# The third batch's norms and scatters a round sooner, both early tiles transposed together, the last batch counted sooner, and the next expert's reads behind the early tiles

## The reference

```python
# 1: gated linear attention, q, k, v, alpha: (4, 8, 768, 48)
for t in range(S):
    state = alpha[:, :, t, :, None] * state + np.einsum('bhd,bhe->bhde', k[:, :, t], v[:, :, t])
    y[:, :, t] = np.einsum('bhd,bhde->bhe', q[:, :, t], state)
x = y as 3072 tokens of 384
# 2: mixture of 8 experts, top 1; w1: (8, 384, 1024), w2: (8, 1024, 384)
logits = (x / (norm(x) + 1e-6)) @ (emb / (norm(emb) + 1e-6)).T / tau
gate_w = softmax(logits) at expert_idx = argmax(logits)
out[mask] = gate_w[mask, None] * (np.maximum(x[mask] @ w1[e], 0.0) @ w2[e])     # for each expert e
# 3: dense network, w_in: (384, 2048), w_out: (2048, 384)
h = x @ w_in
y = np.where(h > 0, h, np.exp(np.minimum(h, 0)) - 1) @ w_out
```

## Time and profile before

| | us |
|---|---|
| median of 3 runs | 927.77 |
| lowest, highest | 925.91, 928.4 |
| profiled execution, own time | 922.87 |
| its span | 921.2 |
| TensorE busy | 886.1 |
| VectorE busy | 435.5 |
| ScalarE busy | 321.7 |
| GpSimd busy | 273.0 |

### The profile page before, as it was taken

How to read it: one execution, slowest core, us unless ns; L and a number is a source line. 1 busy time by engine, 2 the same in 40 slices (tenths; PEclk the granted TensorE clock), 3 DMA queues, 4 the chain that set the end, 5 groups by cost and what they waited for, 6 DMA issues and landing times. The chain is left out here.

```text
span 921.2 us, 16309 instructions
## 1 busy us (share of the span) xinstructions
PE 886.1 (96%) x5729; PEld 779.3 (85%) x5729; DVE 435.5 (47%) x837; ACT 321.7 (35%) x708; POOL 273.0 (30%) x277
## 2 busy tenths in 40 slices
PE   7999999968999999999998999999999999999995
PEld 4777788757989899898997899999999999989994
DVE  6788787863222322223224545445445445445442
ACT  3556656622222222223222223223233223323221
POOL 2212444643576555635816400101001001001001
PEclk8999999979999999999999999999999999999998
DMA  9877875558768797775815301001001001000000
GB/s 151 122 132 120 167 134 107 202 176 274 267 210 283 241 336 251 203 239 150 249 32 163 121 1 44 26 1 52 18 1 61 9 0 66 4 1 35 1 1 34
DMA packets 140975, 107.92 MB, mean 117 GB/s; under 512 B 103354, under 2 KB 129074, under 8 KB 140898
## 3 DMA queue, kind: packets, MB, share of 16 engines
q0 software_dynamic: 25696, 66.09, 22.7%
q1 hardware_dynamic: 115202, 40.79, 21.1%
HBM read 89.51 MB, written 17.35 MB: 116 GB/s over the span
## 5 line engine op out<-in xcount | busy, mean ns | idle before, releaser
L1379 POOL DMA_INDIRECT out<-of,idi x24 | 23.6, 984 | 370.2 <-DVE of L1465 305.5
L1199 PE MATMUL bank<-WX,hdTh 128*128 (+1 forms) x496 | 129.0, 341 | 2.8 <-DVE hdTl L1252 1.6
L1423 PE MATMUL bank<-xT_h,wi_h 128*128 128x512 f32 x288 | 114.1, 396 | 0.0
L1423 PE MATMUL bank<-xT_l,wi_h 128*128 128x512 f32 x288 | 113.6, 394 | 0.0
L1423 PE MATMUL bank<-xT_h,wi_l 128*128 128x512 f32 x288 | 113.3, 394 | 0.0
L1483 ACT ACTIVATE ee<-bank 128x512 f32<-128x512 f32 x96 | 57.5, 598 | 147.3 <-PE bank L1423 144.5
L1505 DVE TENSOR_SCALAR em<-ee 128x512 f32<-128x512 f32 x96 | 44.4, 462 | 136.4 <-ACT ee L1483 134.3
L1120 POOL TENSOR_TENSOR WX<-raw_w,WX 128x3072 fp32r<-128x3072 f32 x14 | 95.7, 6833 | 27.7 <-DMA WX<-moe_w 19.6
L1185 PE MATMUL bank<-WX,xdTh 128*128 (+1 forms) x372 | 100.8, 407 | 1.8 <-issue 1.2
L1486 ACT ACTIVATE g_h<-gg 128x512 fp32r<-128x512 f32 x96 | 60.6, 631 | 116.0 <-DVE gg L1510 114.2
L1514 DVE TENSOR_TENSOR g_l<-gg,g_h 128x512 fp32r<-128x512 f32 x96 | 69.7, 727 | 60.2 <-ACT g_h L1486 59.3
(11 more groups left out here) (210 smaller groups left out, 1449.5 us busy)
## 6 DMA issues: line engine op xcount, KB each, us to landing
WX<-moe_w POOLq DMA_DIRECT2D x14, 1536.0 KB, 10.6
raw_w<-moe_w POOLq DMA_DIRECT2D x14, 1536.0 KB, 8.7
xd<-sorted_x SPq DMA_DIRECT2D x31, 193.0 KB, 6.7
sorted_y<-yd SPq DMA_DIRECT2D x31, 192.5 KB, 4.5
xg<-sorted_y SPq DMA_DIRECT2D x6, 770.0 KB, 4.4
nat_a<-alpha SPq DMA_DIRECT2D x32, 144.0 KB, 3.2
nat_k<-k SPq DMA_DIRECT2D x32, 144.0 KB, 3.2
nat_q<-q SPq DMA_DIRECT2D x32, 144.0 KB
```

Source lines behind the costliest of these rows:

```text
L1199: last = pe.matmul(y_out(t)[:, 0:DM], hdT[a][:, k * P:(k + 1) * P], WX[:, bass.ds(off + (b * WE + KD * F + k * DM), DM)], start=(k == 0 an ...
L1423: last = pe.matmul(bank[4 + i % 2][:, :], a[:, k, w], b[:, k, :], start=(k == 0 and m == 0), stop=(k == KD - 1 and m == 2))
```

## The change

Six things, all of order:

- Batch 2: Ng and Nk move from round 14 into round 13 behind Y0, which itself moves ahead of LA; Ns, Nt and Nr move behind Rr in round 13; Gq to ScalarE's yT0 of round 13. Two of its sums of squares go behind Kt0 and Kt1 of round 13 in place of behind St5. On GpSimd all root steps stand ahead of M1 of round 13 (before, M1 stood behind P2).
- Three of batch 2's scatters stand at the end of round 13's steps, ahead of gam of round 14, and three behind M1 of round 14; before, all six stood behind M1 of round 14.
- Both early tiles' transposes stand ahead of M10u and of the last batch's CT; before, XT(1) stood behind CT.
- Batch 3: NM stands ahead of step W1; step W4 (a quarter subtraction) behind Ro in place of ahead of LA, step W5 behind Nr in place of behind Ro.
- U0 moves from the end of round 15 into the last batch's root steps, behind P0, waits for both early tiles' loads, and now also issues the plain read of expert 1's W1, behind step W1.
- In `po_experts`, the reads of expert 1's W2 stand behind its first lower part.

```diff
-        SOON = ({"LA": ("Rl", "Rx", "Dl")}, {"R": ("Rc", "Rb", "Ro"), "F": ("Rs",), "LA": ("Rn", "Rd", "Y0", "Y1", "Y2", "Y3", "Y4", "Y5", "Y6", "Y7"), "Qh1": ("Rw", "Rp", "Rr")},
-                {"R": ("Ng", "Nk"), "S5": ("Ns", "Nt", "Nr")})
+        SOON = ({"LA": ("Rl", "Rx", "Dl")}, {"R": ("Rc", "Rb", "Ro"), "F": ("Rs", "Rn", "Rd", "Y0"),
+                                             "LA": ("Ng", "Nk", "Y1", "Y2", "Y3", "Y4", "Y5", "Y6", "Y7"),
+                                             "Qh1": ("Rw", "Rp", "Rr", "Ns", "Nt", "Nr")})
...
@@ steps_ve
-                out_ += [("W1", 0), ("NM", PARTIAL), ("W3", 0), ("W4", 0)]
+                out_ += [("NM", PARTIAL), ("W1", 0), ("W3", 0)]
@@ steps_ac
+                elif r == 1 and b == PARTIAL - 1:
+                    for j, name in ((4, "Kt0"), (5, "Kt1")):
+                        out_.insert(place_of(out_, name) + 1, ("SS", b * C + j))
@@ steps_po
                 if b == PARTIAL and r == 0:
-                    out_ += [("PM", b)] + roots + [("SC", b * C + j) for j in range(C)]
+                    out_ += [("PM", b), roots[0], ("U0", 1)] + roots[1:] + [("SC", b * C + j) for j in range(C)]
                 elif b == PARTIAL - 1 and r == 1:
                     i = place_of(out_, "M1")
-                    out_[i + 1:i + 1] = roots[2:]
-                    out_[i:i] = roots[:2]
-                    out_ += [(f"X{i}", b) for i in range(X_STEPS)]
+                    out_[i:i] = roots
+                    out_ += [(f"X{i}", b) for i in range(X_STEPS)] + [("SC", b * C + j) for j in range(HC)]
                 elif b == PARTIAL - 1 and r == 2:
-                    out_ += [("SC", b * C + j) for j in range(C)]
+                    i = place_of(out_, "M1") + 1
+                    out_[i:i] = [("SC", b * C + j) for j in range(HC, C)]
...
-            if n == PAIRS - 1:
-                out_.append(("U0", 1))
@@ pe_a
-                        d(("XT", 0), ("M10u", 0))
+                        d(("XT", 0), ("XT", 1), ("M10u", 0))
@@ po_a, step U0
-                    return upper_load(po, 1, expert_at(po, 1), 0)
+                    for t in range(EARLY):
+                        po.wait_ge(s_xd[t], 16)
+                    e = expert_at(po, 1)
+                    upper_load(po, 1, e, 0)
+                    po.wait_ge(s_w, 1)
+                    return raw_load(po, e, 0, s_raw)
@@ po_experts
-            e = expert_at(po, 1)
-            for x in range(2):
-                po.wait_ge(s_w, 1 + x)
-                if x:
-                    upper_load(po, 1, e, x)
-                else:
-                    po.wait_ge(s_xd[EARLY], 16)
-                raw_load(po, e, x, s_raw)
+            po.wait_ge(s_w, 2)
             for k in range(1, E):
                 for x in range(2):
                     lower_part(po, k, x)
+                    if k == 1 and x == 0:
+                        po.wait_ge(s_xd[EARLY], 16)
+                        e = expert_at(po, 1)
+                        upper_load(po, 1, e, 1)
+                        raw_load(po, e, 1, s_raw)
```

More of the change, by code:

```diff
@@ L290, in build @@
                 {"R": ("Rp", "Rr"), "S5": ("Ng", "Nk"), "LA": ("Ns", "Nt", "Nr")})
-        SOON = ({"LA": ("Rl", "Rx", "Dl")}, {"R": ("Rc", "Rb", "Ro"), "F": ("Rs",), "LA": ("Rn", "Rd", "Y0", "Y1", "Y2", "Y3", "Y4", "Y5", "Y6", "Y7"), "Qh1": ("Rw", "Rp", "Rr")},
-                {"R": ("Ng", "Nk"), "S5": ("Ns", "Nt", "Nr")})
-        LAST = ({"LA": ("Rl", "Rx", "Dl", "N0", "Rc", "Rb", "Ro", "W5", "Rs", "Rn", "Rd", "Rw", "Rp", "Rr", "Rz", "Ng", "Nk", "Ns", "Nt", "Nr", "W6")},)
+        SOON = ({"LA": ("Rl", "Rx", "Dl")}, {"R": ("Rc", "Rb", "Ro"), "F": ("Rs", "Rn", "Rd", "Y0"),
+                                             "LA": ("Ng", "Nk", "Y1", "Y2", "Y3", "Y4", "Y5", "Y6", "Y7"),
+                                             "Qh1": ("Rw", "Rp", "Rr", "Ns", "Nt", "Nr")})
+        LAST = ({"LA": ("Rl", "Rx", "Dl", "N0", "Rc", "Rb", "Ro", "W4", "Rs", "Rn", "Rd", "Rw", "Rp", "Rr", "Rz", "Ng", "Nk", "Ns", "Nt", "Nr",
+                        "W5", "W6")},)
         ROUTE_VE = [SLOW] * (BATCHES - 2) + [SOON, LAST]
         ROUTE_PE = [({}, {"Ta0": ("CT",)})] * (BATCHES - 1) + [({"YN1": ("CT",)},)]
-        ROUTE_AC = [({}, {}, {"Ln0": ("Gq",)})] * (BATCHES - 2) + [({}, {}, {"Ln0": ("Gq",)}), ({"Ln1": ("SL", "Gq")},)]
+        ROUTE_AC = [({}, {}, {"Ln0": ("Gq",)})] * (BATCHES - 2) + [({}, {"yT0": ("Gq",)}), ({"Ln1": ("SL", "Gq")},)]
         ROUTE_PO = [({"Zm": ("ID",)},)] * BATCHES
@@ L1570, in _ @@
             pe_a(pe, d)
-            d(("XT", 1), ("M10", 0), ("M11", 0), ("M10", 1), ("HT0", 0), ("HT1", 0))
+            d(("M10", 0), ("M11", 0), ("M10", 1), ("HT0", 0), ("HT1", 0))
             d(("M11", 1), ("M2", 0), ("HT0", 1), ("HT1", 1), ("M2", 1), ("XT", 2))
```

## The result

| | before | after |
|---|---|---|
| median of 8 runs each, on one chip | 927.62 us (924.79 to 928.92) | 931.69 us (929.98 to 934.68) |
| profiled execution: own time, span | 922.87, 921.2 us | 933.01, 931.4 us |
| granted clock, mean | 0.987 | 0.988 |

The ratio is 1.0051, with a 95% interval from 1.0034 to 1.0067: the changed kernel is **slower**, by 4.1 us between the medians. Forecast were 923.6 us and a gain of 4.2; the range ended at 926.8. The prediction was wrong in sign.

A forecast was written before the change was run, and what follows sets the result against it. TensorE, busy 96% of the span, was taken as the bound, with late early tiles costing 6.36 us through VectorE's chain. 6.36 - 1.0 (W1) - 1.15 (norm) = 4.2 us gain, to 923.6 us; 80% range 920.9 to 926.8.

The forecast's parts named there:

- paragraph on the expert loop: Expert 1's first lower part runs near 202, reads for the second near 210; both over 4.2 us sooner, so neither becomes late.
- part 4: Expert 1's reads placed inside GpSimd's norm chain for the last batch; claimed a cost of 1.15 us, bounds 0 and 2.5.
- The gain term, 6.36 us: VectorE's two stops before tile 0's hdTl, 4.02 us for xdTh and 2.34 for the counts, would go: 6.36 us.
- W1, +1.0 us: Expert 0's W1 read lands behind three more scatters, 1.5 us later, issued 0.5 sooner: net +1.0, bounds -0.5 and +2.0.
- The norm behind the reads, 1.15 us: Last batch's norm on GpSimd, queued behind expert 1's reads, reaches VectorE 0.5 to 1.5 us late; 1.15 taken.
- Rival (a): TensorE's waits near 200 for relu and hdTl drop its clock to half speed: gain 1.0, 926.8 us; chance 0.13.
- Rival (b): GpSimd too slow in rounds 13 and 14, masks late behind norm steps and scatters: gain 1.6, 926.2 us; chance 0.11.
- Rival (c): Early tiles, ahead of the last batch's norm in GpSimd's queue, land late: 928.9 or 931.4 us; chance 0.06.
- the signs that were to show it right: No early-tile wait, tiles by 183.5, last scatter by 176, W1 copy and Ng a microsecond late, hdTl near 201, clock 1.00 through 184-216.
- the signs of its being wrong: Attention ending after 186, P8 out by 191.9 (gain 5 or more), clock 0.50 after 200, early tiles landing after 185.
- parts 1 to 3: Third batch's norms and scatters a round sooner, both early tiles transposed together, last batch counted sooner (worth nothing by itself).

The follow-up runs named there:

- experiment 4: Kernel before with only the new places of expert 1's reads and its first lower part right behind the last scatter: 927.80 us, ratio 1.0053.
- experiments 10 and 11: On a fourth chip, the changed kernel unedited, 932.16 us, and the changed kernel with GpSimd's first expert 1 subtraction waiting for VectorE's whole ladder, 924.56 us.
- kernel 3: Changed kernel with expert 1's reads and first lower part put back where the kernel before has them: 919.68 us, ratio 0.9965.
- experiment 1: Kernel before, unedited, traced again on the second chip: 921.51 us, beside a median of 922.86 there.
- experiment 9: Kernel before, unedited, run and traced on the fourth chip: 926.29 us.
- experiment 6: Changed kernel with expert 1's reads put back and all six third-batch scatters behind round 14's mask, against the kernel before: 925.97 us, ratio 1.0002.
- kernel 2: Changed kernel plus one wait: GpSimd starts expert 1's first lower part only after VectorE's whole ladder; 921.27 us, ratio 0.9986.

## Why the prediction was wrong

**The step that failed** is in its paragraph on the expert loop: "the first runs at about 202, right behind the last scatter", and from it "neither can become late". It asked of the moved subtraction only whether its result comes in time, and not what runs beside it in the new place. Before, it stood at 225.20, beside a VectorE step of the loop that takes one operand from PSUM (`bank`), and the next one at 233.89 beside three more; none was held (VectorE, then GpSimd, in the kernel before):

```profile
229.65 0.56 DVE L1247 TENSOR_TENSOR xdTl<-bank,xdTh 128x384 fp32r<-128x384 f32 x1 [4.51 <-ACT xdTh L1225]
...
234.19 1.29 DVE L1252 TENSOR_TENSOR hdTl<-bank,hdTh 128x512 fp32r<-128x512 f32 x2 [0.39 <-ACT hdTh L1231]
```

```profile
233.89 6.82 POOL L1120 TENSOR_TENSOR WX<-raw_w,WX 128x3072 fp32r<-128x3072 f32 x1 [0.42 <-DMA raw_w<-moe_w]
```

That trace seemed to say that this subtraction harms no one. In its new place it stands beside a ladder of steps on SBUF alone, with hdTl of tile 1 queued behind them. Still, the rows for the question were at hand. The prediction had used the lock for GpSimd's small steps beside VectorE's subtractions and never turned it round. At the 202 that it forecast for the subtraction, with hdTl at 200.8, the steps behind hdTl would have met it just so; 6.82 us beside a ladder that TensorE waits for at 212.10 was the number to put there, as a rival on the slow side. The runs show 7.41 and 7.43 us for a step of 0.15 to 0.17, a loss of 4.9 us for part 4 alone (experiment 4) and 7.6 for the one wait (experiments 10 and 11).

The Trainium skill has the rule and a detail that fits: SBUF — State Buffer, Who interferes with whom, says that an elementwise step with a scalar operand (`tensor_scalar`) can take the port pair that VectorE shares with GpSimd although it has one SBUF input, that two SBUF inputs meet GpSimd's reads, and that whoever comes second is blocked for the whole instruction and not slowed. The traces agree on who is held: it was a TENSOR_SCALAR in three executions and a SCALAR_TENSOR_TENSOR with two SBUF inputs in a fourth, and each ended within 0.05 us of GpSimd's end. On who comes second they don't, by the recorded starts: VectorE's stands 0.64 to 0.66 us ahead of GpSimd's. They show too that hdTl and xdTl, with one input from PSUM, ran beside such a subtraction at their usual length, as did a copy of one number on each partition from SBUF to SBUF (`yd<-xd`, 0.15 us each time, five times in the trace of the kernel before). That the shared ports are what holds the step is the page's explanation; the runs show the exclusion, not its seat.

**The gain term, 6.36 us,** was read rightly in the early tempo (4.02 + 2.34), and there the runs give 5.5 of it: hdTl of tile 0 comes 14.7 us after the attention's end in kernel 3 (201.12 - 186.42) and 20.3 in experiment 1 (204.05 - 183.80). In the late tempo the two stops were 4.08 us, and less the norm, some 1.5, that would be 2.6; hdTl comes 15.8 to 15.9 us after the attention's end in the changed kernel's three traces and 17.8 in experiment 9 (208.48 - 190.67), 1.9 to 2.0 us sooner. The profiled execution, 4.9 us under the median of the runs, could have warned: it stood for executions that the median didn't. The forecast took the same gain off both.

**W1, +1.0 us,** was mis-sized. Its two parts were 1.5 us for three scatters more in front of the read's end and -0.5 for a read issued sooner. The read was issued no sooner (164.8 against 164.4), and the delay was 2.5 us in kernel 3: nearly the upper end's "five of them in full", without its discount. The copy started 2.9 us later (179.36 against 176.50) and the attention ended 2.6 us later (186.42 against 190.16 - 6.36 = 183.80); 0.4 of both stood already in round 12 (147.39 against 147.03), and the 2.3 to 2.5 that are left are beyond the bound of +2.0. In the late tempo the delay was 1.2 us (experiment 6), near the forecast's 1.5 for three scatters. (The paragraph on W1 also misreads a row: beside its 403 GB/s the DMA share is 1.03, not 1.06; nothing hangs on it.)

**The norm behind the reads, 1.15 us,** was right: 1.61 in the changed kernel's first trace, 1.46 to 1.48 in the four later ones with all parts, 0.83 with part 4 alone, none with the reads put back. **Rival (a)**, that the clock takes it back after waits of 2 us, was right as a mechanism: where TensorE waits 2.2 to 2.4 us for the relu and as long again for hdTl of tile 0 (two traces of the changed kernel, both of kernel 2), the clock is at 0.50 soon behind the second wait; in the changed kernel's third trace it is so behind the first, of 2.19 us. With one wait of 1.75 us, and 0.83 before it (kernel 3), it stays at 1.00. It cost some 1.6 us. **Rival (b)**, a mask of round 14 late by the scatters, may have taken a microsecond in the late tempo (the 1.7 us of experiment 6); in the early one no such wait is in the traces. **Rival (c)**, tiles too late for the norm, didn't happen: they had landed 2.6 us after their issue.

Of the signs that were to show it right, no wait for the tiles and the norm's late microsecond came in the changed kernel, and the last scatter by 176 (174.87) and hdTl near 201 (201.12) in kernel 3, in the tempo of the forecast. In kernel 3 the early tiles landed near 186, not by 183.5 (issued at 180.7 and 181.8, 4.5 to 5.1 us each); TensorE didn't wait for them, because its attention ended late as well, at 186.42. Of the signs of its being wrong three came: the attention past 186, a clock of 0.50 after 200, and tiles landing after 185. The signs looked no further than tile 0's hdTl but for the clock; the loss is behind it.

The sum, by the traces of the second chip: parts 1 to 3 are worth 5.5 us (of the early tempo) less 2.3 for W1, 3.3 us before rounding, measured 3.2. With part 4's norm and the clock (1.46 + 1.6) 0.2 us remain, measured 1.6 (experiment 2); no trace accounts for the difference, and kernel 2's traced execution was itself 1.4 us above its median. With the lock it is a loss, measured 4.1, 5.8 and 5.8 on three chips.

## What to carry to other kernels

When a long GpSimd instruction on SBUF is moved, ask what VectorE runs beside it in the new place, and who waits for the end of that: here one step of some 0.16 us was held for the instruction's whole length, and everything queued behind it with it. A place where the same instruction harmed no one says nothing if the neighbours there are of another kind (one input from PSUM, in this case). One wait that orders the two engines gave back 7.6 us, and TensorE never waited for what it put off; a second look at what is still waited for (hdTl), on top of parts 1 to 3, brought 4.4 us, about what the change had been meant to give. And before two traces are subtracted, align them on a stretch with the same instructions: 4.6 us of the first pair's difference weren't the change's.

## What the runs showed of the hardware that was not expected

- A VectorE step of 0.15 to 0.17 us took 7.41 to 7.43 us beside a GpSimd subtraction of 6.73 to 6.75 us over 128x3072. By the records it began some 0.65 us ahead of GpSimd's start and was still the one held. The step kth, held in three traces, took its 0.17 us in experiment 4, where it began 1.04 us ahead of GpSimd's start (204.25 and 205.29).
- The same attention, instruction for instruction, runs in two tempos 4 to 5 us apart, which part in rounds 7 to 12, at ScalarE's first state copy. In these runs it went with the chip or the loading (four traces of four on one chip early, eight of eight on two others late, one of each on the first). The cause stays open.
- Six scatters of 193 KB, three of them issued within 4 us behind a read of 2 x 1.5 MB in engines that are full (about 400 GB/s), delayed its first half by 2.1 to 2.5 us in one tempo and 1.2 in the other, against four scatters issued later.
